# The low part of g in the dense layers: three of sixteen blocks made at another place in VectorE's order

## The chip, the core and the metric

The kernel runs on one core of a Trainium2 chip. The metric is the device time of one execution in microseconds. The engines are named as in the profile: PE (TensorE, matrix products; PEld is its weight loads), DVE (VectorE), ACT (ScalarE), POOL (GpSimd) and SP (SyncE, which issues DMAs here). Each works through its own list of instructions in order and waits on semaphores for the others.

## What is computed

Three parts in a row. Attention over 4 x 8 heads of 576 positions, once pooled by 4 and once in a narrow band; its output, reshaped, is x with 2304 tokens of 512 numbers. Two dense layers on x, which are the place of the change:

```python
h = x @ w_in                                  # 2304x512 @ 512x2048
g = np.where(h >= 1, h, np.where(h <= -1, 0.0, (h + 1) ** 2 / 4))
y = g @ w_out                                 # 2304x2048 @ 2048x512
```

Then a layer of 8 experts with a capacity of 288 tokens each, to which tokens are assigned by sorted gate logits.

## The kernel before

**Products in two parts.** To get fp32 precision, each operand is held as a high part, rounded to the type that PE multiplies, and a low part, the rest. A product is then three matmuls: high x high, high x low, low x high (`pe_halves`, line 528). For g the high part is a copy by ACT (line 640) and the low part a subtraction by DVE (line 669), which therefore has to wait for the copy.

**Chunks and steps.** The dense layers run over 9 chunks of 256 tokens, and each chunk over steps s = 0 to 18. The 2048 hidden features are 16 blocks f of 128. In step s PE makes the hidden block H(s) (12 matmuls, s below 16), and then adds block f = s - 3 to the output (6 matmuls of 512 columns, s from 3 on), for which it waits for the low part of g of that block (semaphore `glo_ready`). So there are three steps at the start with hidden products alone, and three at the end (16, 17, 18) with output products alone. The last chunk has no steps 16 to 18 on PE: after step 15 it takes blocks 13, 14 and 15 for the first half of the tokens and then for the second (`pe_last_products`).

**From H to g.** For block f DVE clamps H(f) to between -1 and 1 (line 660); ACT makes relu(H - 1) (line 633) and then squares the clamped one (line 634); DVE adds the two, which is g (line 665); ACT copies the high part (line 640); DVE subtracts for the low part (line 669). In DVE's list, step s holds the clamp of block s, the sum of block s - 1 and the low part of block s - 2. In ACT's list, step s holds relu and square of block s and the high part of block s - 1.

**What else stands in a step.** In step 0 PE turns the output of the chunk before for the gate logits, in step 1 it makes them, and DVE copies them out (line 556). In step 16 ACT and DVE split the next chunk's x into high (line 610) and low (line 615) parts, four pieces each; H(0) of the next chunk needs them piece by piece. Beside this runs the rest of the attention in units of two heads. Chunk 0 has a plan of its own with three units (`FIRST_PLAN`), chunks 1 to 4 have two units each (a loop), chunk 5 one, chunks 6 and 7 (a loop) and 8 none. A unit is spread over steps by `PLAN`: `turn` (PE turns q and k; ACT copies q; DVE copies k, line 372, and pools both over 4, lines 377 and 383), `scores`, two steps later the sums, `turn_p` (DVE copies a part of the turned probabilities, line 424) and `out` (PE makes the unit's output, lines 315 and 324; ACT copies its pooled part od, line 363; DVE adds both into xT, line 432). In chunks 1 to 4 `turn` of the first unit stands in step 1 and `out` of the second in step 16; in chunk 0 `turn_p` of its last unit stands in step 16 and `out` in 17. Chunk 0 also brings in the weights in pieces (ACT line 690, DVE line 707). POOL scales probabilities (lines 458, 465) and pools v.

In DVE's list the unit's instructions come last in a step, behind the instructions on g and the split of x.

```python
PLAN = [dict(turn=1, scores=3, turn_p=7, out=8), dict(turn=9, scores=11, turn_p=15, out=16)]
FIRST_PLAN = [dict(turn=None, scores=None, turn_p=1, out=2), dict(turn=3, scores=5, turn_p=9, out=10),
              dict(turn=11, scores=12, turn_p=16, out=17)]
```

Of the kernel before, what the change touches and what calls it, by code (L numbers as in the profile page):

```python
# [4 lines left out]
F32 = mybir.dt.float32  # L5
# [4 lines left out]
ALU = mybir.AluOpType  # L10
# [22 lines left out]
FC = FF // 128  # L33
# [3 lines left out]
RING = 4  # L37
# [29 lines left out]
def network(nc, q, k, v, w_in, w_out, w_gate, w1, w2, out, xt_dram, y_dram):  # L67
# [4 lines left out]
    with whole:  # L72
        def sem(name):
            return whole.enter_context(nc.semaphore(name))


        logits = whole.enter_context(nc.sbuf_tensor("logits", [128, YT + TILES, E], F32))
        ident = whole.enter_context(nc.sbuf_tensor("ident", [128, 128], F32))
        PS = whole.enter_context(nc.psum_tensor("PS", [128, 8, 512], F32))
        bank = [PS[:, i, :] for i in range(8)]  # L80

        con = {}
        for name, shape, dt in (("thr", [128, DIG, MOST], F32),
                                ("rev", [128, E], F32),
                                ("slot", [128, GP], F32),
                                ("weight", [128, DIG, TILES], F32),
                                ("three", [128, GT], F32),
                                ("tile_no", [128, TILES], F32),
                                ("part_no", [128, 1], F32),
                                ("alive", [128, TILES], F32),  # L90
                                ("zero", [128, TILES], F32),
                                ("unit", [128, DIG, 128], BF16),
                                ("below", [128, 128], BF16),
                                ("ones", [128, 128], BF16)):
            con[name] = whole.enter_context(nc.sbuf_tensor(name, shape, dt))
        made = sem("made")
        dense_layers(nc, sem, PS, bank, ident, logits, con, made, qf, kf, vf, w_in, w_out, w_gate, xt_dram, y_dram)
        experts(nc, sem, bank, ident, logits, con, made, w1, w2, y_dram, out)
# [8 lines left out]
def dense_layers(nc, sem, PS, bank, ident, logits, con, made, qf, kf, vf, w_in, w_out, w_gate, xt_dram, y_dram):  # L107

    ctx = ExitStack()
    with ctx:  # L110
        def sb(name, shape, dt=F32):
            return ctx.enter_context(nc.sbuf_tensor(name, shape, dt))
# [42 lines left out]
        c_sb = scratch[:, 3, 0:2 * CT].rearrange("p (a t) -> p a t", a=2)  # L155
        r_sb = scratch[:, 3, 2 * CT:4 * CT].rearrange("p (a t) -> p a t", a=2)
# [4 lines left out]
        g_sb = sb("g_sb", [128, 2, CT])  # L161
        g = [sb(f"g{s}", [128, RING, CT], F32R) for s in range(2)]
# [21 lines left out]
        h_ready, c_ready, r_ready, q_ready, g_ready = sem("h_ready"), sem("c_ready"), sem("r_ready"), sem("q_ready"), sem("g_ready")  # L184
        ghi_ready, glo_ready, g_used = sem("ghi_ready"), sem("glo_ready"), sem("g_used")
# [322 lines left out]
        def dve_units(dve, c, plan, s):  # L508
            for at, n, k, b in units_of(c, plan):
                if s == at["turn"]:  # L510
                    dve_kT(dve, n, TM)
                    dve_pool_k(dve, n)
                    dve_pool_q(dve, n)
                if s == at["scores"]:
                    dve_mask(dve, n, TM)
                    dve_dtop(dve, n, TM)
                if at["scores"] is not None and s == at["scores"] + 2:
                    dve_rden(dve, n, TM)
                    dve_rdend(dve, n)
                if s == at["turn_p"]:  # L520
                    dve_pT(dve, n, TM)
                if s == at["out"]:
                    dve_xT(dve, n, TM)
# [26 lines left out]
        def dve_yT(dve, c):  # L550
            dve.wait_ge(y_turned, YT * c + 2)
            dve.tensor_copy(yT[:, 1, :, :].rearrange("p k m -> p (k m)"), A[1][:, :]).then_inc(yT1_ready, 1)

        def dve_logits(dve, c):
            dve.wait_ge(lg_ready, c + 1)
            dve.tensor_copy(logits[:, ds(YT * c, YT), :].rearrange("p a e -> p (a e)"), A[2][:, 0:YT * E]).then_inc(lg_out, 1)
# [55 lines left out]
        def dve_split_x(dve, c):  # L612
            for kk in range(KC):
                dve.wait_ge(xs_hi, KC * c + kk + 1)
                dve.tensor_tensor(xs[1][:, kk, :], xload[:, kk, :], xs[0][:, kk, :].bitcast(F32),
                                  ALU.subtract).then_inc(xs_lo, 1)
# [9 lines left out]
        def act_chunk(act, c, units, first=False, more=True):  # L626
# [23 lines left out]
            act.wait_ge(y_stored, 16 * YT * c + 16)  # L650
            act.activation(y_sb[:, 0, :], Y[0][:, :], ACT.Copy).then_inc(y0_out, 1)

        def dve_chunk(dve, c, units, first=False, more=True):
            for s in range(STEPS):
                if first and s == FIRST_PLAN[0]["turn_p"]:
                    dve_units(dve, c, units, s)
                if s < FC:
                    dve.wait_ge(h_ready, FC * c + s + 1)
                    dve.wait_ge(g_ready, FC * c + s + 1)
                    dve.tensor_scalar(c_sb[:, s % 2, :], H[s % 2][:, 0:CT], -1.0, 1.0, ALU.max, ALU.min).then_inc(c_ready, 1)  # L660
                f = s - 1
                if 0 <= f < FC:
                    dve.wait_ge(q_ready, FC * c + f + 1)
                    dve.wait_ge(glo_ready, FC * c + f + 1)
                    dve.tensor_tensor(g_sb[:, f % 2, :], c_sb[:, f % 2, :], r_sb[:, f % 2, :], ALU.add).then_inc(g_ready, 1)  # L665
                f = s - 2
                if 0 <= f < FC:
                    dve.wait_ge(ghi_ready, FC * c + f + 1)
                    dve.tensor_tensor(g[1][:, f % RING, :], g_sb[:, f % 2, :], g[0][:, f % RING, :].bitcast(F32),  # L669
                                      ALU.subtract).then_inc(glo_ready, 1)  # L670
                if s == 0 and not first:
                    dve_yT(dve, c)
                if s == 1 and not first:
                    dve_logits(dve, c)
                if s == FC and more:
                    dve_split_x(dve, c + 1)
                if not first or s != FIRST_PLAN[0]["turn_p"]:
                    dve_units(dve, c, units, s)
                if first and s in CHUNK_PIECES:
                    dve_piece(dve, CHUNK_PIECES[s])  # L680
            dve.wait_ge(y_ready, YT * c + 2)
            dve.wait_ge(y_stored, 16 * YT * c + 16)
            dve.tensor_copy(y_sb[:, 1, :], Y[1][:, :]).then_inc(y1_out, 1)
# [20 lines left out]
        def dve_piece(dve, i):  # L704
            c = slice(ORDER[i] * PIECE, (ORDER[i] + 1) * PIECE)
            dve.wait_ge(piece_hi, i + 1)
            dve.tensor_tensor(W[1][:, c], scratch[:, SLOT_OF[i], :], W[0][:, c].bitcast(F32), ALU.subtract).then_inc(piece_lo, 1)

        with nc.Block() as block:  # L709
# [232 lines left out]
            def _(dve):  # L942
# [26 lines left out]
                dve_rdend(dve, EARLY)  # L969
                dve.wait_ge(mask_ready, 1)  # L970
                dve_chunk(dve, 0, FIRST_PLAN, first=True)
                with dve.Fori(1, MIXED) as c:
                    dve_chunk(dve, c, PLAN)
                dve_chunk(dve, MIXED, PLAN[0:1])
                dve.wait_ge(con_ready, 7)
                for i in range(1, DIG):
# [762 lines left out]
```

## Time and profile before

| | |
|---|---|
| time, median of 3 runs | 876.4 us (876.13, 876.4, 880.44) |
| profiled execution, first to last instruction | 876.4 us |
| PE busy | 825.6 us, 94% |
| PE weight loads | 747.9 us, 85% |
| DVE busy | 509.4 us, 58% |
| ACT busy | 406.7 us, 46% |
| POOL busy | 332.7 us, 38% |
| low part of g (DVE, line 669) | 144 instructions, 70.0 us |
| sum g (DVE, line 665) | 144 instructions, 63.0 us |
| high part of g (ACT, line 640) | 144 instructions, 58.5 us |

The attention's first units take the first 56 us, the dense layers (with the other units beside them) run from 56 to 569 us, and routing and experts from there to the end. The page's chain of work that ended last holds 34% of the span in all, and all its pieces lie behind 569 us. A busy PE is not a PE at its peak: its records overlap, so a delay shows both as idle time and as a longer group. In the timelines, a number in brackets is the idle time of the engine before that instruction and what ended it.

### The profile page before, as it was taken

The numbers are of one execution on the slowest core, as the hardware profiler recorded it, in microseconds if no ns is written. First come the engines' busy times: TensorE is split into PE (matmuls) and PEld (weight loads), VectorE is DVE, ScalarE is ACT, GpSimd is POOL, SyncE is SP. The second block draws the span as 40 slices with busy tenths as digits, with TensorE's granted clock in tenths as the row PEclk, the third lists the DMA queues.
The fourth block names the chain that finished last, engine by engine and source line by source line (L and its number), as shares of the span: only waits on it lengthen the run. The fifth ranks groups of instructions, "written<-read, shape, count | busy, mean of one in ns | idle before, by whom it ended". The sixth has DMA issues, their size and how long they took to land. (4 is left out here: it accounts for less than half of the span.)

```text
span 876.4 us, 21162 instructions
## 1 busy us (share of the span) xinstructions
PE 825.6 (94%) x7658; PEld 747.9 (85%) x7658; DVE 509.4 (58%) x1424; ACT 406.7 (46%) x1006; POOL 332.7 (38%) x391
## 2 busy tenths in 40 slices
PE   6979999999999999999999999939999999999995
PEld 4867888888888888888998989838999999999995
DVE  4668766655755665563434344376766766756620
ACT  4655555444534444553444444304455454454461
POOL 6661133203311331240000000007776786787782
PEclk9899999999999999999999999958999999999998
DMA  9975521321322223201101000005624625615511
GB/s 199 255 194 136 142 67 42 94 80 27 79 79 63 57 79 79 66 1 39 50 1 48 0 24 2 24 21 201 220 95 163 231 64 187 227 46 217 204 53 45
DMA packets 99301, 85.49 MB, mean 98 GB/s; under 512 B 63664, under 2 KB 71856, under 8 KB 99248
## 3 DMA queue, kind: packets, MB, share of 16 engines
q1 hardware_dynamic: 93808, 74.74, 29.7%
q0 software_dynamic: 3072, 9.44, 3.7%
q10 hardware_dynamic: 2368, 0.59, 0.4%
q8 instruction: 34, 0.56, 0.3%
q14 instruction: 19, 0.16, 0.1%
HBM read 70.60 MB, written 14.16 MB: 97 GB/s over the span
## 5 line engine op out<-in xcount | busy, mean ns | idle before, releaser
L528 PE MATMUL PS<-xs,W 128*128 128x256 f32 x1728 | 234.1, 285 | 1.3 <-DVE xT L432 1.3
L528 PEld LDWEIGHTS PS<-xs,W 128*128 128x128 f32 x1728 | 222.6, 189 | 12.4 <-issue 3.3
L528 PE MATMUL PS<-W,g 128*128 128x512 f32 x864 | 223.9, 396 | 5.3 <-DVE g L669 5.0
L528 PEld LDWEIGHTS PS<-W,g 128*128 128x128 f32 x864 | 152.5, 188 | 37.4 <-DVE g L669 9.7
L633 ACT ACTIVATE scratch<-PS,minus 128x256 f32<-128x256 f32 x144 | 68.1, 473 | 218.7 <-DVE scratch L660 218.7
L660 DVE TENSOR_SCALAR scratch<-PS 128x256 f32<-128x256 f32 x144 | 61.0, 423 | 124.4 <-PE PS L528 123.9
L441 POOL TENSOR_TENSOR P<-P,top 128x640 f32<-128x640 f32 x11 | 13.9, 1261 | 224.8 <-DVE top L391 224.8
L1539 POOL TENSOR_TENSOR w1s<-w1r,w1s 128x512 fp32r<-128x512 f32 x64 | 80.7, 1287 | 28.2 <-ACT w1s L1427 27.9
L1334 PE MATMUL PS<-exs,w1s 128*128 128x288 f32 x256 | 81.1, 317 | 0.0
L1334 PE MATMUL PS<-ehs,w2s 128*128 128x288 f32 x256 | 80.8, 316 | 0.0
L1335 PE MATMUL PS<-exs,w1s 128*128 128x288 f32 x256 | 76.0, 297 | 0.0
L1336 PE MATMUL PS<-exs,w1s 128*128 128x288 f32 x256 | 75.7, 296 | 0.0
L1335 PE MATMUL PS<-ehs,w2s 128*128 128x288 f32 x256 | 75.5, 295 | 0.0
L1336 PE MATMUL PS<-ehs,w2s 128*128 128x288 f32 x256 | 75.2, 294 | 0.0
L1571 POOL TENSOR_TENSOR w2s<-w2r,w2s 128x512 fp32r<-128x512 f32 x56 | 71.7, 1291 | 9.2 <-ACT w2s L1465 8.8
L634 ACT ACTIVATE scratch<-scratch,half 128x256 f32<-128x256 f32 x144 | 72.0, 500 | 0.0
L669 DVE TENSOR_TENSOR g<-g_sb,g 128x256 fp32r<-128x256 f32 x144 | 70.0, 486 | 0.1
L1616 POOL MEMSET full<- 128x8 bf16 x1 | 0.1, 109 | 178.0 <-POOLq L709 178.0
L665 DVE TENSOR_TENSOR g_sb<-scratch 128x256 f32<-128x256 f32 x144 | 63.0, 437 | 1.2 <-ACT scratch L634 1.1
L640 ACT ACTIVATE g<-g_sb 128x256 fp32r<-128x256 f32 x144 | 58.5, 407 | 1.4 <-DVE g_sb L665 1.4
L1461 ACT ACTIVATE ehs<-PS 128x288 fp32r<-128x288 f32 x64 | 26.3, 411 | 57.7 <-PE PS L1336 57.5
L1334 PEld LDWEIGHTS PS<-exs,w1s 128*128 128x128 f32 x256 | 48.9, 191 | 0.4
(198 smaller groups left out, 1433.3 us busy)
## 6 DMA issues: line engine op xcount, KB each, us to landing
w1r<-in_moe_w SPq DMA_DIRECT2D x16, 1024.0 KB, 5.1
w2r<-in_moe_w SPq DMA_DIRECT2D x16, 1024.0 KB
vd<-in_v SPq DMA_DIRECT2D x16, 288.0 KB
xt<-xT SPq DMA_DIRECT2D x16, 288.0 KB, 2.2
y<-scratch SPq DMA_DIRECT2D x18, 256.0 KB, 2.2
vw<-in_v SPq DMA_DIRECT2D x34, 128.0 KB, 2.8
scratch<-in_moe_w_in SPq DMA_DIRECT2D x8, 512.0 KB, 5.9
scratch<-in_moe_w_out SPq DMA_DIRECT2D x8, 512.0 KB, 4.8
```

Of the source, the lines that this page charges most:

```text
L528: r = pe.matmul(psum, wsel(w[i]), xsel(x[j]), start=first and t == 0, stop=last and t == 2)
L633: act.activation(r_sb[:, s % 2, :], H[s % 2][:, 0:CT], ACT.Relu, bias=minus[:, :]).then_inc(r_ready, 1)
L634: act.activation(c_sb[:, s % 2, :], c_sb[:, s % 2, :], ACT.Square, bias=half[:, :], scale=0.5).then_inc(q_ready, 1)
L640: act.activation(g[0][:, f % RING, :], g_sb[:, f % 2, :], ACT.Copy).then_inc(ghi_ready, 1)
L660: dve.tensor_scalar(c_sb[:, s % 2, :], H[s % 2][:, 0:CT], -1.0, 1.0, ALU.max, ALU.min).then_inc(c_ready, 1)
L665: dve.tensor_tensor(g_sb[:, f % 2, :], c_sb[:, f % 2, :], r_sb[:, f % 2, :], ALU.add).then_inc(g_ready, 1)
L669: dve.tensor_tensor(g[1][:, f % RING, :], g_sb[:, f % 2, :], g[0][:, f % RING, :].bitcast(F32), ALU.subtract).then_inc(glo_ready, 1)
L1334: pe.matmul(psum, wh, xh, start=first, stop=False)
L1335: pe.matmul(psum, wh, xl, start=False, stop=False)
L1336: return pe.matmul(psum, wl, xh, start=False, stop=last)
L1539: pool.tensor_tensor(w1s[1][:, :, c], w1r[:, :, c], w1s[0][:, :, c].bitcast(F32), ALU.subtract).then_inc(w1_lo, 1)
L1571: pool.tensor_tensor(w2s[1][:, f, :], w2r[:, f, :], w2s[0][:, f, :].bitcast(F32), ALU.subtract).then_inc(w2_lo, 1)
```

## The change

The sum and the low part of g become two small functions, `dve_g` and `dve_g_rest`, with the waits that they had. In DVE's list three of the sixteen low parts of each chunk stand elsewhere:

- block 0: in step 1, behind the sum of block 0 and the copy of the logits, ahead of the unit's instructions of that step (before: in step 2, behind the sum of block 1);
- block 14: in step 16, now ahead of the sum of block 15 (before: right behind it);
- block 15: in step 16, behind the sum of block 15 and ahead of the split of x and of the unit's instructions (before: in step 17).

The other thirteen, and the lists of the other engines, are as before; no instruction is added or taken away.

```diff
--- before.py
+++ after.py
@@ -650,6 +650,16 @@
             act.wait_ge(y_stored, 16 * YT * c + 16)
             act.activation(y_sb[:, 0, :], Y[0][:, :], ACT.Copy).then_inc(y0_out, 1)
 
+        def dve_g(dve, c, f):
+            dve.wait_ge(q_ready, FC * c + f + 1)
+            dve.wait_ge(glo_ready, FC * c + f + 1)
+            dve.tensor_tensor(g_sb[:, f % 2, :], c_sb[:, f % 2, :], r_sb[:, f % 2, :], ALU.add).then_inc(g_ready, 1)
+
+        def dve_g_rest(dve, c, f):
+            dve.wait_ge(ghi_ready, FC * c + f + 1)
+            dve.tensor_tensor(g[1][:, f % RING, :], g_sb[:, f % 2, :], g[0][:, f % RING, :].bitcast(F32),
+                              ALU.subtract).then_inc(glo_ready, 1)
+
         def dve_chunk(dve, c, units, first=False, more=True):
             for s in range(STEPS):
                 if first and s == FIRST_PLAN[0]["turn_p"]:
@@ -658,20 +668,20 @@
                     dve.wait_ge(h_ready, FC * c + s + 1)
                     dve.wait_ge(g_ready, FC * c + s + 1)
                     dve.tensor_scalar(c_sb[:, s % 2, :], H[s % 2][:, 0:CT], -1.0, 1.0, ALU.max, ALU.min).then_inc(c_ready, 1)
-                f = s - 1
-                if 0 <= f < FC:
-                    dve.wait_ge(q_ready, FC * c + f + 1)
-                    dve.wait_ge(glo_ready, FC * c + f + 1)
-                    dve.tensor_tensor(g_sb[:, f % 2, :], c_sb[:, f % 2, :], r_sb[:, f % 2, :], ALU.add).then_inc(g_ready, 1)
-                f = s - 2
-                if 0 <= f < FC:
-                    dve.wait_ge(ghi_ready, FC * c + f + 1)
-                    dve.tensor_tensor(g[1][:, f % RING, :], g_sb[:, f % 2, :], g[0][:, f % RING, :].bitcast(F32),
-                                      ALU.subtract).then_inc(glo_ready, 1)
+                if s == FC:
+                    dve_g_rest(dve, c, FC - 2)
+                if 1 <= s <= FC:
+                    dve_g(dve, c, s - 1)
+                if s == FC:
+                    dve_g_rest(dve, c, FC - 1)
+                if 3 <= s < FC:
+                    dve_g_rest(dve, c, s - 2)
                 if s == 0 and not first:
                     dve_yT(dve, c)
                 if s == 1 and not first:
                     dve_logits(dve, c)
+                if s == 1:
+                    dve_g_rest(dve, c, 0)
                 if s == FC and more:
                     dve_split_x(dve, c + 1)
                 if not first or s != FIRST_PLAN[0]["turn_p"]:
```

## Rows read from the trace of the kernel before

A row of a timeline gives start (us), length (us), engine, line and operation, output and inputs, and the number of instructions merged into it. A row of waits gives the engine and line that waited, what released it, and then total, count and longest.

**Rows 1.** Busy time by stretch; then granted TensorE clock, DMA share, GB/s

```profile
56.00:566.00 510.00, 502.08 (x4180) 446.23 (x4180) 288.43 (x685) 243.99 (x645) 87.34 (x140) 1.00 0.21 58
600.00:606.00 6.00, 6.00 (x48) 5.92 (x47) 2.78 (x8) 1.54 (x5) 6.00 (x6) 0.55 0.86 298
```

**Rows 2.** Waits of PE over the span: total us, times, longest us

```profile
PE PS L528 <- DVE g L669: 5.0, 11, 1.2
```

**Rows 3.** Timeline of PE, two undisturbed steps of a chunk: start us, length us

```profile
484.75 1.59 PE L528 MATMUL PS<-xs,W 128*128 128x256 f32 x12
486.18 1.54 PE L528 MATMUL PS<-W,g 128*128 128x512 f32 x6
487.56 1.59 PE L528 MATMUL PS<-xs,W 128*128 128x256 f32 x12
```

**Rows 4.** Timeline of PE, first block of chunk 4

```profile
312.19 3.12 PE L528 MATMUL PS<-xs,W 128*128 128x256 f32 x24
315.71 1.67 PE L528 MATMUL PS<-W,g 128*128 128x512 f32 x6 [0.39 <-DVE g L669]
```

**Rows 5.** Timeline of all engines at 310 us, start of chunk 4

```profile
310.84 0.41 ACT L640 ACTIVATE g<-g_sb 128x256 fp32r<-128x256 f32 x1
...
311.40 0.17 DVE L556 COPY logits<-PS 128x16 f32 x1 [1.04 <-PE PS L543]
...
312.45 0.76 DVE L372 COPY kT<-PS 128x576 f32<-128x576 f32 x1 [0.87 <-PE PS L249]
```

**Rows 6.** Timeline of all engines at 299 us, end of chunk 3, with a unit's output

```profile
299.69 0.41 ACT L640 ACTIVATE g<-g_sb 128x256 fp32r<-128x256 f32 x1
...
300.44 1.43 DVE L615 TENSOR_TENSOR xs<-scratch,xs 128x256 fp32r<-128x256 f32 x4 [0.74 <-ACT xs L610]
...
302.42 3.42 PE L528 MATMUL PS<-W,g 128*128 128x512 f32 x12
...
303.70 0.42 DVE L669 TENSOR_TENSOR g<-g_sb,g 128x256 fp32r<-128x256 f32 x1
```

**Rows 7.** Timeline of all engines at 464 us, end of chunk 6, without units

```profile
463.15 4.37 PE L528 MATMUL PS<-W,g 128*128 128x512 f32 x18
...
464.71 0.43 DVE L665 TENSOR_TENSOR g_sb<-scratch 128x256 f32<-128x256 f32 x1 [0.27 <-ACT scratch L634]
465.05 0.42 DVE L669 TENSOR_TENSOR g<-g_sb,g 128x256 fp32r<-128x256 f32 x1
465.25 0.42 ACT L640 ACTIVATE g<-g_sb 128x256 fp32r<-128x256 f32 x1 [0.26 <-DVE g_sb L665]
...
466.01 1.43 DVE L615 TENSOR_TENSOR xs<-scratch,xs 128x256 fp32r<-128x256 f32 x4 [0.54 <-ACT xs L610]
...
467.83 1.66 PE L528 MATMUL PS<-W,g 128*128 128x512 f32 x6 [0.31 <-DVE g L669]
```

**Rows 8.** Timeline of all engines at 561 us, end of the last chunk

```profile
561.30 0.42 DVE L665 TENSOR_TENSOR g_sb<-scratch 128x256 f32<-128x256 f32 x1 [0.27 <-ACT scratch L634]
561.64 0.99 DVE L669 TENSOR_TENSOR g<-g_sb,g 128x256 fp32r<-128x256 f32 x2
...
562.11 3.28 PEld L528 LDWEIGHTS PS<-W,g 128*128 128x128 f32 x15 [0.50 <-DVE g L669]
```

**Rows 9.** Timeline of all engines at 70 us, start of chunk 0

```profile
70.32 0.82 DVE L432 TENSOR_TENSOR xT<-PS,od 128x348 f32<-128x348 f32 x2 [0.76 <-ACT od L363]
```

**Rows 10.** Timeline of all engines at 117 us, end of chunk 0

```profile
116.70 1.65 POOL L465 TENSOR_TENSOR Pd<-Pd,rdend 72x288 f32<-72x288 f32 x2
116.94 0.88 DVE L669 TENSOR_TENSOR g<-g_sb,g 128x256 fp32r<-128x256 f32 x1
...
119.55 0.41 DVE L424 COPY pT<-PS 128x256 f32<-128x256 f32 x1
...
120.63 1.37 PE L315 MATMUL PS<-pT,vw 64*64 64x58 f32 x40
```

**Rows 11.** Timeline of PE, first products of chunk 0

```profile
56.21 4.50 PE L528 MATMUL PS<-xs,W 128*128 128x256 f32 x24 [1.30 <-DVE xT L432]
```

## The prediction

> **What bounds the kernel now.** I read four views, in this order. Busy time by stretch: between 56 and 566 us, the dense layers, PE is busy for 502.1 of 510 us at a granted clock of 1.00 (2.4 GHz), DVE for 288 [rows 1]. So in this stage only what makes PE wait counts, and there are 8 us of PE idle to win at all. The chain that ended last is of no use here: it reaches back only to the routing, behind the dense stage. The waits of PE: of that idle, 5.0 us in 11 pieces end with the low part of g (line 669), the longest 1.2 [rows 2]. Then the timelines around those pieces. The reader should see in them the order in which DVE works, for each of the waits ends with an instruction that DVE could have run earlier.
>
> How to price one piece. An undisturbed step is 12 hidden products (from 484.75 to 486.18, 1.43 us) and 6 output products (to 487.56, 1.38 us); a group starts 0.16 us before the one ahead of it has ended, and six output products take 1.54 us [rows 3]. So an idle of i shown on PE is a delay of i + 0.16, and the group behind a wait is longer (1.67 for 1.54), since its first weight load was not done ahead [rows 4]. A piece costs **i + 0.29 us**.
>
> **Term 1, the first block (f = 0), five chunks with units (1 to 5).** The low part of g for f = 0 was made in step 2, behind the unit's copy of kT and both poolings: PE, which ended H(2) and H(3) at 315.31, starts the output products at 315.71, idle 0.39, released by it [rows 4]. Now it is made in step 1, behind the logits copy and ahead of kT. Its input, the high part, is done at 310.84 + 0.41 = 311.25, before the logits copy starts (311.40), and DVE sits idle from 311.57 to 312.45, until PE has turned k [rows 5]. An instruction of 0.42 us fits there with some 0.4 to spare: the move costs nothing, and the wait it adds (on the high part) is already met; behind it on DVE stand kT and the poolings, with PE's scores behind those, but not even they move. If that cover were gone, kT, the poolings and clamp(2) would come 0.34 later (the next instruction starts that long after one of these, 465.05 behind 464.71 [rows 7]). The output products of f = 0 then follow H(3) at once. What is late next is PE itself. Gain: 5 x (0.39 + 0.29) = **3.4 us**. The three chunks without units show no such wait and gain nothing here.
>
> **Term 2, the last block (f = 15), four chunks (1 to 4) that end with a unit's output.** Step 17 makes the low part of f = 15 at 303.70, behind the split of x and behind xT, and xT waits for ScalarE's copy of od. PE shows no idle but a stretched group: 12 output products take 3.42 us, where 1.67 + 1.38 = 3.05 would do [rows 3, 4, 6]. Now DVE makes it as soon as ScalarE has the high part, 299.69 + 0.41 = 300.10, some 3.5 us sooner. g(15) comes one instruction later (0.34), but ScalarE is at pdT until 299.7 and picks it up hardly later; the split starts at about 300.5 instead of 300.44, and xT waits for od until 302.96 anyway [rows 6]. Gain: 4 x 0.37 = **1.5 us**.
>
> **Term 3, the last block, three chunks (5 to 7) without a unit at the end.** There g(15) ran at 464.71 and the low part of f = 14 at 465.05, right when its high part came. The new order puts g(15) behind that: 465.05 + 0.34 = 465.39, 0.68 later. ScalarE starts the high part of f = 15 0.54 behind g(15): 465.93, done 466.35; the low part runs from 466.40 to 466.82, and the wait it adds for that high part is where DVE idles, some 0.7 us, with the split behind it. PE wants it at about 467.36, 0.16 before the end of its group (463.15 + 4.37 = 467.52), so 0.5 us are to spare, where today it starts at 467.83 [rows 7]. The split, behind it, ends near 468.1 instead of 467.44; H(0) of the next chunk needs its first quarter at 468.7 and the last one 1.1 us later. Gain: 3 x (0.31 + 0.29) = **1.8 us**. The count fits: 5 + 3 pieces here and in term 1 make 2.9 us of idle, and the other 3 of the 11, with 2.1 us and the longest, are in chunk 0 at blocks that the change does not move [rows 2].
>
> **Term 4, the last chunk, a loss.** With no H left and the products ordered by token tile, PE takes f = 13, 14, 15 with three products each, so that it wants f = 15 at 562.11 + 0.13 + 3 x 0.23 = 562.93. Today the low part of f = 15 ends at 561.64 + 0.99 = 562.63 and no one waits for it. Now g(15) waits for the low part of f = 14 (which can't start before 561.64): 561.98 instead of 561.30. ScalarE starts 0.54 behind it, ends at 562.94, the low part ends at 563.40, and PE starts at 563.45: 0.52 + 0.13, **0.6 us lost** [rows 7, 8]. The move that wins in term 3 loses here, since PE comes one and a half groups sooner.
>
> **Term 5, chunk 0.** At its start the low part of f = 0 is no longer in step 2, but what PE does behind that block, the turn of the next unit, waits for xT, which ends at 71.14 and depends on PE and ScalarE alone: 0 [rows 9]. At its end a unit's turn_p falls into step 16, so now pT's copy on DVE (119.55 to 119.96) comes behind the wait for the high part of f = 15. POOL works until 118.35, and DVE's two-input subtraction beside it takes 0.88 instead of 0.42 [rows 10]. With slow ones: low(14) to about 117.5, g(15) to 118.3, low(15) from 118.8, split to 120.4, pT to 120.8; PE, which starts the unit's output at 120.63, would wait 0.2 us. With none slow it waits 0; with every one of the seven instructions 0.46 longer than the quick ones, near 1.0. I take the slow rows that stand there: **0.3 us lost**, bounds 0 and 1.0.
> The Trainium skill, GPSIMD Engine Reference, section Key points, says that GpSimd shares its SBUF interfaces with VectorE and that they contend when the DVE instruction has two SBUF inputs; that speaks against queueing three such instructions in a row ahead of the split. The trace agrees where POOL runs (0.88 for 0.42), and by the rule as by the row the sum is the same as long as POOL rests at the ends of chunks 1 to 8.
>
> **Sum.** -3.4 - 1.5 - 1.8 + 0.6 + 0.3 = -5.8 us. The profiled execution spans 876.4 us and the median of the runs is 876.4, so the sum is made against both alike: **870.6 us**. No instruction, byte or DMA is added, and SP's and POOL's queues keep their order. Everything behind the dense stage moves forward as a block. A measurement of this kernel can tell about 0.5%, 4.4 us, from no change.
>
> **Rivals.**
> A. As computed: 870.6, own range 869.5 to 872.0. Chance 0.63.
> B. The gains are partly given back: the waits move on to the next thing that DVE or ScalarE owes (r of a block, P of a unit through POOL). For it speaks that five of the gains come right ahead of a unit's scores; against it, that DVE is busy for only 288 of the 510 us [rows 1]. With term 1 halved and term 2 lost: 870.6 + 1.7 + 1.5 = 873.8. Chance 0.15.
> C. The clock at the start of the experts. At 600 to 606 us the granted clock is 0.55, though PE is busy throughout [rows 1]. The dense stage ends sooner, so the stretch can lie otherwise over the first expert products. Its price from rows: 24 hidden products took 4.50 us at 56 us, begun at the lower level (1.2 GHz), and 3.12 at the higher one, a difference of 1.4 [rows 4, 11]. Either sign: 872.0 (chance 0.07) or 869.2 (0.05).
> D. It does not do what it says: PE is held by its own sequencer behind these semaphores and the gaps stay; terms 4 and 5 remain: 876.4 + 0.9 = 877.3. Chance 0.04. Against it: line 669 at 303.70 ends at 304.12, inside the stretched group [rows 6].
> E. Slower: the split of x becomes what ends last. From low(14) to the last quarter there are seven two-input instructions; if POOL ran beside all, each took 0.46 longer, 3.2 us in all, against a slack of 1.7 (468.1 against 468.7 + 1.1). It decides from a delay of 1.7 us on. Over by 1.5 us at the eight chunk ends ahead of another chunk it costs 12 us: 882.6; it takes four such ends to use up the 5.8. For it speaks the slow row in chunk 0 [rows 10]; against it, that POOL has no units left at the ends of chunks 5 to 7. Chance 0.06.
>
> **How the numbers follow.** The likeliest is A. Faster by over 0.5% (below 872.0): A but its tail, half of C: 0.66. Within: B, D, the rest of A and C: 0.28. Slower: E: 0.06. The range takes in A, C and B: 869.1 to 874.6.
>
> **What would show it.** After the change PE's waits on line 669 fall from 11 to about 4 (three in chunk 0, one or two in the last chunk); the groups behind H(3) in chunks 1 to 5 start 0.16 before its end; the 12 products at a chunk's end take 3.05; the last chunk shows a new wait of about 0.4; pT of chunk 0 ends near 120.8. Wrong would be: a wait of PE for the split of x, or a later kT copy.

## The result, and the profile after

| | before | after |
|---|---|---|
| median of 6 runs each | 877.1 us (875.7 to 880.4) | 873.1 us (872.4 to 875.4) |
| ratio after / before, 95% interval | | 0.9943 [0.9922, 0.9964] |
| profiled execution | 876.4 us | 873.6 us |

The change makes the kernel 0.57% faster, 5.0 us of 877, with an interval from 3.2 to 6.8 us. The ratio is not that of the two medians, which lie 4.0 us apart. Forecast were 5.8 us. The interval holds it, and the measured median lies within the forecast range of 869.1 to 874.6.

The waits of PE for the low part of g went from 5.0 us in 11 pieces [rows 2] to this (line 660 is now the low part, 656 the sum), in the view of waits of PE of the kernel after: total, count, longest.

```profile
PE PS L528 <- DVE g L660: 1.5, 4, 0.6
```

Not all of that fall is the change's. Three of the pieces lie in chunk 0, at blocks that the change does not move: they add up to 2.2 us before and to 1.2 here, where 8.2 us of chunk 0 ran at half clock (the granted clock at 0.5, 1.2 GHz) instead of 3.1. When the same kernel ran again (e0_again below) they were 2.2 again, and all waits for the low part 2.5 us in 4 pieces.

In the view of busy time by stretch, PE idles 5.4 of the 510 us between 56 and 566 us, where it idled 7.9 [rows 1]; the granted clock is 0.99. The dense stage ends at 562.1 now (565.9 before), so the last 4 us of this window belong to what follows it.

```profile
56.00:566.00 510.00, 504.59 (x4208) 451.53 (x4204) 291.39 (x689) 245.74 (x648) 87.30 (x143) 0.99 0.21 59
```

What follows is the same place as in rows 4 and 5, the start of chunk 4, in the timeline of all engines of the kernel after. The high part (line 640) is done at 310.34, the low part runs at 310.60 between the logits copy and kT, and the copy of kT waits for PE as before. The output products start at 314.26, 0.16 before the hidden ones end (311.30 + 3.12), with no wait, and take 1.55 instead of 1.67.

```profile
309.94 0.40 ACT L640 ACTIVATE g<-g_sb 128x256 fp32r<-128x256 f32 x1
...
310.51 0.17 DVE L556 COPY logits<-PS 128x16 f32 x1 [1.04 <-PE PS L543]
310.60 0.41 DVE L660 TENSOR_TENSOR g<-g_sb,g 128x256 fp32r<-128x256 f32 x1
...
311.30 3.12 PE L528 MATMUL PS<-xs,W 128*128 128x256 f32 x24
311.56 0.76 DVE L372 COPY kT<-PS 128x576 f32<-128x576 f32 x1 [0.54 <-PE PS L249]
...
314.26 1.55 PE L528 MATMUL PS<-W,g 128*128 128x512 f32 x6
```

The end of chunk 3, as in rows 6: the low part of block 15 is ahead of the split, the split starts 0.34 behind it, and twelve output products take 3.04 us, where it was 3.42.

```profile
299.28 0.42 ACT L640 ACTIVATE g<-g_sb 128x256 fp32r<-128x256 f32 x1
...
299.73 0.43 DVE L660 TENSOR_TENSOR g<-g_sb,g 128x256 fp32r<-128x256 f32 x1 [0.56 <-ACT g L640]
...
300.07 1.43 DVE L615 TENSOR_TENSOR xs<-scratch,xs 128x256 fp32r<-128x256 f32 x4
...
301.88 3.04 PE L528 MATMUL PS<-W,g 128*128 128x512 f32 x12
```

The end of chunk 6, as in rows 7. The low part of block 14 at 461.86, then the sum of block 15, ACT's high part 0.53 later, the low part of block 15 at 463.18, the split. PE goes on without a wait.

```profile
461.42 0.40 ACT L640 ACTIVATE g<-g_sb 128x256 fp32r<-128x256 f32 x1
461.86 0.42 DVE L660 TENSOR_TENSOR g<-g_sb,g 128x256 fp32r<-128x256 f32 x1 [0.57 <-ACT g L640]
462.20 0.42 DVE L656 TENSOR_TENSOR g_sb<-scratch 128x256 f32<-128x256 f32 x1
462.73 0.42 ACT L640 ACTIVATE g<-g_sb 128x256 fp32r<-128x256 f32 x1 [0.91 <-DVE g_sb L656]
...
463.18 0.43 DVE L660 TENSOR_TENSOR g<-g_sb,g 128x256 fp32r<-128x256 f32 x1 [0.56 <-ACT g L640]
463.52 1.42 DVE L615 TENSOR_TENSOR xs<-scratch,xs 128x256 fp32r<-128x256 f32 x4
...
465.58 1.59 PE L528 MATMUL PS<-xs,W 128*128 128x256 f32 x12
```

The end of the last chunk, as in rows 8. Here the same order leaves PE idle at 559.10, until the low part that began at 558.62 has ended.

```profile
557.38 0.42 DVE L660 TENSOR_TENSOR g<-g_sb,g 128x256 fp32r<-128x256 f32 x1 [0.58 <-ACT g L640]
557.72 0.42 DVE L656 TENSOR_TENSOR g_sb<-scratch 128x256 f32<-128x256 f32 x1
...
558.17 0.42 ACT L640 ACTIVATE g<-g_sb 128x256 fp32r<-128x256 f32 x1 [0.83 <-DVE g_sb L656]
558.62 0.43 DVE L660 TENSOR_TENSOR g<-g_sb,g 128x256 fp32r<-128x256 f32 x1 [0.48 <-ACT g L640]
...
559.10 2.12 PE L528 MATMUL PS<-W,g 128*128 128x512 f32 x8 [0.27 <-DVE g L660]
```

And the end of chunk 0, as in rows 10. The sum, beside POOL, takes 0.89, but the low part of block 14 ahead of it takes 0.43, and the split is as quick as elsewhere (1.42 for four), and pT's copy ends at 122.50, in time for the unit's output.

```profile
119.03 0.89 DVE L656 TENSOR_TENSOR g_sb<-scratch 128x256 f32<-128x256 f32 x1
...
120.75 1.42 DVE L615 TENSOR_TENSOR xs<-scratch,xs 128x256 fp32r<-128x256 f32 x4
...
122.09 0.41 DVE L424 COPY pT<-PS 128x256 f32<-128x256 f32 x1
...
122.76 1.37 PE L315 MATMUL PS<-pT,vw 64*64 64x58 f32 x40
```

**Where the time went.** One number per chunk says more than the total. It is the time from the first hidden product of a chunk to that of the next (in the last, to the last output product), read from the starts of line 528 in the timeline.

| us | ahead | 0 | 1 | 2 | 3 | 4 | 5 | 6 | 7 | 8 | behind |
|---|---|---|---|---|---|---|---|---|---|---|---|
| before | 56.2 | 67.87 | 60.56 | 60.53 | 60.51 | 60.53 | 54.76 | 48.36 | 48.30 | 47.80 | 310.9 |
| after | 58.2 | 68.00 | 59.50 | 59.55 | 59.51 | 59.55 | 53.59 | 47.68 | 47.75 | 48.41 | 311.9 |
| after less before | +2.0 | +0.1 | -1.1 | -1.0 | -1.0 | -1.0 | -1.2 | -0.7 | -0.6 | +0.6 | +1.0 |

The nine chunks are 5.7 us shorter. The two stretches around them, whose instructions the change does not touch, are 3.0 longer in this pair of executions, which is why the profiled executions differ by 2.8 us alone. The 2.0 ahead go with the clock: between 0 and 56 us the granted clock is 0.91 before and 0.85 after. In the four of the 14 profiled executions where it is 0.85 to 0.87, the stretch ahead takes 58.2 to 59.6 us; in the ten with 0.88 or more, 56.0 to 57.1. Behind the dense layers both have some 32 us at half clock (32.1 and 32.3), so the 1.0 there does not come from more time at half clock; its cause is open.

### The profile page after: what moved, and what is told of

It is laid out like the page before. It is cut to its first block and busy times, and to the rows that moved or that the text cites. A ratio compares the mean times of both kernels' runs of the same rounds, so it can differ in the third digit from the quotient of the medians.

```text
span 873.6 us, 21162 instructions
## 1 busy us (share of the span) xinstructions
PE 827.0 (95%) x7658; PEld 752.3 (86%) x7658; DVE 509.8 (58%) x1424; ACT 406.9 (47%) x1006; POOL 332.5 (38%) x391
## 5 line engine op out<-in xcount | busy, mean ns | idle before, releaser
L528 PE MATMUL PS<-W,g 128*128 128x512 f32 x864 | 221.4, 394 | 1.5 <-DVE g L660 1.5
```

The costliest lines, as they stand in the source:

```text
L528: r = pe.matmul(psum, wsel(w[i]), xsel(x[j]), start=first and t == 0, stop=last and t == 2)
```

## The experiments

Theory: PE's waits for the low part of g came from VectorE's order alone, and each goes where VectorE gets there earlier. Rivals: B, the gain is given back at the next wait; E, the split of x becomes late. Chunks 1 to 8 repeat to within 0.1 us between executions, so I read them from the trace, and use timed runs for the total. Ratios are to the kernel before on the same chip, in the same session; e4, e5, e6, e10 and e11 have one profiled execution each and no ratio. The diffs are against the changed kernel, where nothing else is said.

| run | 0 | 1 | 2 | 3 | 4 | 5 | 6 | 7 | 8 | sum 1 to 8 | behind |
|---|---|---|---|---|---|---|---|---|---|---|---|
| e0_again | 67.92 | 59.49 | 59.50 | 59.50 | 59.50 | 53.51 | 47.75 | 47.74 | 48.39 | 435.4 | 307.6 |
| e1_first_only | 67.84 | 59.87 | 59.85 | 59.85 | 59.85 | 54.08 | 48.29 | 48.33 | 47.87 | 438.0 | 306.7 |
| e4_behind_turn | 67.97 | 59.91 | 59.91 | 59.85 | 59.86 | 54.09 | 48.29 | 48.32 | 47.86 | 438.1 | 309.8 |
| e2_last_only | 68.25 | 60.19 | 60.20 | 60.20 | 60.20 | 54.25 | 47.71 | 47.70 | 48.32 | 438.8 | 308.2 |
| e3_keep14 | 67.97 | 59.55 | 59.55 | 59.51 | 59.55 | 53.51 | 47.76 | 47.75 | 47.88 | 435.1 | 306.4 |
| e8_swap | 68.02 | 59.49 | 59.50 | 59.50 | 59.50 | 53.52 | 47.71 | 47.75 | 47.88 | 434.8 | 314.3 |
| e5_pad4 | 68.05 | 59.85 | 59.84 | 59.83 | 59.83 | 53.91 | 48.31 | 48.13 | 48.74 | 438.4 | 312.4 |
| e10_pad4_end | 68.79 | 59.50 | 59.50 | 59.50 | 59.55 | 53.63 | 47.99 | 47.75 | 48.38 | 435.8 | 306.8 |
| e6_pad9 | 69.29 | 59.60 | 59.60 | 59.60 | 59.60 | 54.41 | 50.81 | 48.88 | 48.51 | 441.0 | 311.5 |
| e11_pad9_end | 67.91 | 59.52 | 59.55 | 59.51 | 59.55 | 54.43 | 49.25 | 48.84 | 48.43 | 439.1 | 309.5 |
| e7_shift_g | 68.05 | 59.85 | 59.84 | 59.84 | 59.84 | 53.90 | 48.11 | 48.12 | 48.74 | 438.2 | 306.4 |
| e9_shift_xs | 68.34 | 59.60 | 59.60 | 59.60 | 59.60 | 53.70 | 47.99 | 48.01 | 48.15 | 436.2 | 307.2 |

### The changed kernel again

> The changed kernel once more, beside the others of this series. The nine chunks (from the first hidden product of one to that of the next) took 67.9, 60.6, 60.5, 60.5, 60.5, 54.8, 48.4, 48.3, 47.8 us before and 68.0, 59.5, 59.5, 59.5, 59.5, 53.6, 47.7, 47.8, 48.4 after. Theory (the gain lies in the order of VectorE): chunks 1 to 8 repeat to 0.05 us each, sum 435.5 against 441.4; what else differs between runs lies ahead of the dense layers, in chunk 0 and in the experts, and follows the granted clock. Rival (part of the gain is given back behind the dense layers): the stretch behind them is again about 1 us longer than before.

Ratio 0.9947 [0.9933, 0.9961], 870.2 against 875.6 us. Chunks 1 to 8 repeat within 0.08 us each. Behind them it takes 307.6 us, 3.3 less than in the profiled execution of before. That alone does not show that nothing is given back there, for the runs were made on several chips, and this stretch differs by chip: from the first product of the third expert to that of the seventh, one expert takes 33.2 to 33.3 us in the four runs on chip 0 (e0 to e3), 33.3 to 33.4 in the four on chip 11 (e7, e9, e10, e11) and 33.8 in the four on chip 13 (e4, e5, e6, e8), with the same instructions. It took 33.8 in both profiles of the first pair. What speaks to it are the timed ratios, which compare on one chip. Over the eight kernels that have one (the first result, e0, e1, e2, e3, e7, e8, e9) the timed gain is 4.4 us on average and the nine chunks are 4.7 us shorter. In seven of them the chunks' gain lies inside the timed interval, and for this run it stands at the edge (5.9 in the chunks, 3.4 to 5.9 by the ratio). So nothing like the 3.2 us of rival B is given back; a few tenths can't be excluded.

### Block 0 alone

```diff
-                if s == FC:
-                    dve_g_rest(dve, c, FC - 2)
                 if 1 <= s <= FC:
                     dve_g(dve, c, s - 1)
-                if s == FC:
-                    dve_g_rest(dve, c, FC - 1)
-                if 3 <= s < FC:
+                if 3 <= s <= FC + 1:
                     dve_g_rest(dve, c, s - 2)
```

> Only block 0's low part is moved to step 1; blocks 14 and 15 are as before. Theory: chunks 1 to 5 get shorter by 0.66 each, 3.3 us in all, chunks 6 to 8 stay at 48.4, 48.3, 47.8; the total falls by 3.3 us. Rival B (given back): the wait moves on to the unit's scores or to the next low part and less than 0.3 per chunk is left, 1.7 in all or less.

Ratio 0.9957 [0.9943, 0.9972]. Chunks 1 to 5 are shorter by 0.69, 0.68, 0.66, 0.68 and 0.68, 3.4 us in all; 6 to 8 are as before. Rival B would have left less than 0.3 each. It falls for this term.

### Blocks 14 and 15 alone

```diff
-                if 3 <= s < FC:
+                if 2 <= s < FC:
                     dve_g_rest(dve, c, s - 2)
...
-                if s == 1:
-                    dve_g_rest(dve, c, 0)
```

> Only blocks 14 and 15 are moved in step 16; block 0 is as before, in step 2. Theory: chunks 1 to 4 shorter by 0.35 each, 5 to 7 by 0.5 to 0.6 each, 8 longer by 0.6, chunk 0 by 0 to 0.3: together 2.5 us less. Rival B: the next chunk starts no sooner, since its hidden products then wait for the split of x, and nothing is gained in chunks 5 to 7.

Ratio 0.9977 [0.9961, 0.9993]. Chunks 1 to 4 are shorter by 0.37, 0.33, 0.31, 0.33 (1.3 us), 5 to 7 by 0.51, 0.65, 0.60 (1.8 us), and 8 is longer by 0.52. The two halves of the change add up: 3.4 and 2.6 against 6.0 for the whole (e0_again) in chunks 1 to 8.

### Block 14 left behind the sum of block 15

```diff
-                if s == FC:
-                    dve_g_rest(dve, c, FC - 2)
                 if 1 <= s <= FC:
                     dve_g(dve, c, s - 1)
+                if 3 <= s <= FC:
+                    dve_g_rest(dve, c, s - 2)
                 if s == FC:
                     dve_g_rest(dve, c, FC - 1)
-                if 3 <= s < FC:
-                    dve_g_rest(dve, c, s - 2)
```

> As the changed kernel, but in step 16 the low part of block 14 stays behind the sum of block 15; only block 15's is moved ahead of the split of x. Theory: the wait that the changed kernel has in the last chunk comes only from block 14 standing ahead of the sum, so chunk 8 falls back from 48.4 to 47.8, and all others stay at 59.5 (1 to 4), 53.6, 47.7, 47.8; 0.6 us less than the changed kernel in all. Rival (the two low parts in a row are what delays it): chunk 8 stays at 48.4.

Chunk 8 falls to 47.88, the others stay. In the timeline of all engines of this kernel the sum is back at 0.34 ahead of the low part of block 14, both low parts (x2) have ended at 559.35, and PE's products wait for none of them. What is left is the wait of the weight loads (PEld) for block 14, 0.50 as before the change [rows 8]; the changed kernel had 0.47 there and another 0.71 for block 15.

```profile
558.02 0.43 DVE L656 TENSOR_TENSOR g_sb<-scratch 128x256 f32<-128x256 f32 x1 [0.27 <-ACT scratch L634]
558.36 0.99 DVE L660 TENSOR_TENSOR g<-g_sb,g 128x256 fp32r<-128x256 f32 x2
558.48 0.42 ACT L640 ACTIVATE g<-g_sb 128x256 fp32r<-128x256 f32 x1 [0.18 <-DVE g_sb L656]
558.84 3.30 PEld L528 LDWEIGHTS PS<-W,g 128*128 128x128 f32 x15 [0.50 <-DVE g L660]
```

So the loss in the last chunk came from block 14 standing ahead of the sum, and no chunk needs it there. By its trace this version beats both kernels, by 0.5 us over the changed one in chunk 8; its ratio of 0.9932 [0.9911, 0.9953] overlaps with the 0.9947 of the changed one, so timing alone doesn't tell them apart.

### Block 0 in step 1, but behind the unit

```diff
-                if s == 1:
-                    dve_g_rest(dve, c, 0)
...
                 if not first or s != FIRST_PLAN[0]["turn_p"]:
                     dve_units(dve, c, units, s)
+                if s == 1:
+                    dve_g_rest(dve, c, 0)
```

(and blocks 14 and 15 as before)

> Only block 0's low part is moved to step 1, but to its end, behind the unit's copy of kT and the poolings. Theory (PE waited only since the low part stood behind clamp(2) and the sum of block 1, about 0.7 us of VectorE's work): it then ends at about 315.0 on the time base of before, ahead of H(3)'s end at 315.3, and chunks 1 to 5 get shorter by 0.66 each, as with the place ahead of the unit. Rival (the place ahead of the poolings is what matters): at most half of it, 0.3 each. In chunk 0 it stands ahead of the weight piece as in the other.

Chunks 1 to 5 are as with the place ahead of the unit, to 0.06 us. The timeline of all engines of this kernel, start of chunk 4, shows why: the low part at 313.44, ahead of the clamp, ends 0.3 us before the hidden products (311.06 + 3.11 = 314.17), and the output products follow at once.

```profile
311.06 3.11 PE L528 MATMUL PS<-xs,W 128*128 128x256 f32 x24
...
313.44 0.42 DVE L660 TENSOR_TENSOR g<-g_sb,g 128x256 fp32r<-128x256 f32 x1
313.77 0.42 DVE L670 TENSOR_SCALAR scratch<-PS 128x256 f32<-128x256 f32 x1
...
314.02 1.55 PE L528 MATMUL PS<-W,g 128*128 128x512 f32 x6
```

What PE had waited for were the clamp and the sum that stood ahead of it, 0.7 us, not the poolings. The place ahead of the poolings is free, but it isn't what brings the gain.

### How late may the split of x be?

One instruction more on VectorE between the low part of block 15 and the split, in chunks 1 to 7:

```diff
                 if s == FC:
                     dve_g_rest(dve, c, FC - 1)
+                    if more and not first:
+                        dve.tensor_reduce(spare[:, :], g_sb[:, 0:1, :].to_broadcast([128, 4, CT]), AX.X, ALU.add)
```

with 9 in the place of 4 in the second pair. In e5 and e6 `spare` was allocated ahead of g, in e10 and e11 behind g.

> The changed kernel with one more instruction on VectorE between the low part of block 15 and the split of x in chunks 1 to 7: a sum over 4 x 256 elements, about 1.1 us, whose result nobody uses. It asks for the slack of the split. After the change the first piece of the split ends at 463.94 and PE takes it at 465.35 in chunk 6, 1.4 us of slack. Theory: nothing is lost, chunks 5 to 7 stay at 53.6, 47.7, 47.8. Rival E (the split ends last from a small delay on): they get longer by up to 1.1 each.

> The same with 9 x 256 elements, about 2.5 us. Theory: at the ends of chunks 5 to 7 the split is then late by 2.5 - 1.4 = 1.1 and the restart adds 0.1, so each gets longer by 1.1 to 1.3 us; chunks 1 to 4, where PE has a unit's output to make before, stay at 59.5 (slack there some 3.5 us). Rival E would have 2.5 each in all seven; no effect at all would mean that the hidden products do not hang on it.

e5 was a miss: every chunk from 1 to 8 was longer by 0.3 to 0.6 us than in e0_again, the last one too, which has no such instruction. A late split can't do that. But the output products came every 0.2334 us instead of 0.2291. The new tensor of 4 numbers ahead of g had moved g by 32 bytes. In e6 the shift was 64 bytes, the pace 0.2301, and the chunks behind the late splits were longer, but in chunk 6 by more than a late split explains (below). Hence both again at the old address:

> As the run with the sum over 4 x 256 elements ahead of the split of x, but the unused result lies behind all other tensors, so that g starts at the same SBUF address as in the changed kernel. In the first try, where it lay ahead of g and moved it by 32 bytes, the output products came every 0.2334 us instead of 0.2291, which made all chunks longer. Theory: at the old address the pace is 0.2291 again and the inserted 1.1 us costs nothing: chunks 59.5 (1 to 4), 53.6, 47.7, 47.7, 48.4. Rival (VectorE's extra instruction itself slows PE): 59.8, 53.9, 48.3, 48.1, 48.7 as in the first try.

> The same for the sum over 9 x 256 elements, 2.5 us. Theory: the split is late by 2.5 - 1.4 = 1.1 us at the ends of chunks 5, 6 and 7 alone; these get longer by 1.1 to 1.3 us each (the next chunk's first product comes later) and chunks 1 to 4 stay at 59.5. A stretch at half clock behind such a wait, as the first try showed one behind chunk 5, would come on top.

e10: 1.1 us more ahead of the split cost nothing measurable in chunks 1 to 4, 7 and 8, and 0.12 in chunk 5. Chunk 6 has 0.24 more. Half of it lies at its gate logits, whose 16 products take 1.95 us instead of the 1.85 of e0_again; the other half I have no cause for. Chunk 0, which has no such instruction, has 0.9 more, with a stretch of 6.8 us at half clock near its start. e11: chunks 1 to 4 stay, 5 to 7 are longer by 0.92, 1.50 and 1.10, 3.5 us in all. In its timeline of all engines, end of chunk 5, the inserted sum takes 2.55 us, the split starts at 417.04, 2.46 behind it, and PE waits for it, idle 0.64 (plus the overlap of 0.16 and the unprefetched start).

```profile
414.23 0.43 DVE L661 TENSOR_TENSOR g<-g_sb,g 128x256 fp32r<-128x256 f32 x1 [0.48 <-ACT g L641]
414.58 2.55 DVE L679 TENSOR_REDUCE spare<-g_sb 128x9 f32<-128x2304 f32 x1
...
417.04 1.42 DVE L616 TENSOR_TENSOR xs<-scratch,xs 128x256 fp32r<-128x256 f32 x4
...
417.51 1.70 PE L529 MATMUL PS<-xs,W 128*128 128x256 f32 x12 [0.64 <-DVE xs L616]
```

So the slack of the split at these ends lies between 1.1 and 2.5 us. The waits for it at the ends of chunks 5, 6 and 7 are 0.64, 0.61 and 0.80 us. Priced as before (plus 0.29) that is 0.9, 0.9 and 1.1 lost, and the slack is 2.46 - 0.64 - 0.16, some 1.7 us (1.5 at the end of chunk 7), not the 1.4 of the expectation. The rest of chunk 6's 1.50 is a second wait that the late split brings with it: at 421.81 the gate logits' products wait 0.29 us for ACT's copy (line 549), which they do not in e0_again. Rival E's mechanism is real, but the change is 1.5 us or more away from it.

### The address of g alone

```diff
+        shift = sb("shift", [128, 8])
         g = [sb(f"g{s}", [128, RING, CT], F32R) for s in range(2)]
```

> The changed kernel with 32 unused bytes ahead of the two tensors of g, and nothing else: they start at 220832 and 224928 instead of 220800 and 224896, a multiple of 32 but not of 64. Theory of the address: output products every 0.2334 instead of 0.2291 us, 96 of them in a chunk, 0.3 to 0.4 us longer per chunk and 3 us in all. Rival (the first try's slower pace came with its extra instruction or was that execution's own): 0.2291 and the chunks of the changed kernel.

Ratio 0.9973 [0.9954, 0.9991], where the changed kernel without the shift had 0.9947 [0.9933, 0.9961]; the intervals overlap, so the chunks have to tell. Chunks 1 to 8 add up to 438.2 against 435.4. The view of groups by line, of the changed kernel again and of this one: 864 output products, busy time and mean.

```profile
L528 PE MATMUL PS<-W,g 128*128 128x512 f32 x864 | 221.3, 394 | 2.5 <-DVE g L660 2.5
```

```profile
L529 PE MATMUL PS<-W,g 128*128 128x512 f32 x864 | 224.2, 397 | 2.5 <-DVE g L661 2.5
```

Their start to start is 0.2333 us. So the address is shown as the cause of e5's miss; what in the memory makes it so is not. The same with x, in the version with block 14 left in its place (e3_keep14):

```diff
+        shift = sb("shift", [128, 8])
         xs = [sb(f"xs{s}", [128, KC, CT], F32R) for s in range(2)]
...
+        shift_g = sb("shift_g", [128, 8])
         g = [sb(f"g{s}", [128, RING, CT], F32R) for s in range(2)]
```

> The version that keeps block 14 behind the sum of block 15, with the two parts of x moved by 32 bytes from 210464 to 210496, from a multiple of 32 to one of 64, and g by 64 bytes, which keeps it a multiple of 64. If the address of what PE streams or loads matters for its pace, the hidden products may come faster than every 0.1195 us (1728 of them: 0.001 each is 1.7 us). Rival: no difference; chunks 59.5, 53.5, 47.75, 47.75, 47.9 as without the shift.

The hidden products came every 0.1193 instead of 0.1196 us, but the output products every 0.2317 instead of 0.2293; chunks 1 to 8 take 436.2 against the 435.1 of e3_keep14. Ratio 0.9941 [0.9922, 0.9960]. Nothing was won with these two shifts together; x alone was not moved. "A multiple of 64" is not the rule either, since g stood on one here. It is not g's address alone, for in e6_pad9 g stood at the same one (64 bytes on) and the pace was 0.2301. What differed there was the place of x, the order of block 14 and the inserted sum.

### Chunk 0: the low part ahead of the sum where PE waits

Against e3_keep14:

```diff
+                swapped = first and s in (4, 6, 15)
+                if swapped:
+                    dve_g_rest(dve, c, s - 2)
                 if 1 <= s <= FC:
                     dve_g(dve, c, s - 1)
-                if 3 <= s <= FC:
+                if 3 <= s <= FC and not swapped:
                     dve_g_rest(dve, c, s - 2)
```

> As the version that keeps block 14 behind the sum of block 15, and in chunk 0, steps 4, 6 and 15, the low part of the earlier block stands ahead of the sum of the later one. These are the three steps of chunk 0 where PE waited for a low part before and still waits (0.2 to 1.2 us idle each). Theory: each of these waits shrinks by 0.34 us, chunk 0 by up to 1.0 us (less where its start runs at half clock), the others as in the version without it: 47.8 in chunk 8, total 0.6 to 1.6 us under the changed kernel. Rival (the sum's delay pushes ScalarE's high part, which makes the next low part late): chunk 0 does not get shorter.

A miss: chunk 0 took 68.02 us, no less than without it (67.97). Ratio 0.9924 [0.9905, 0.9943], not to be told from 0.9932. In its timeline of PE two of the three waits for the low part are gone, and one is 0.33:

```profile
77.92 1.63 PE L528 MATMUL PS<-W,g 128*128 128x512 f32 x6 [0.33 <-DVE g L660]
...
85.22 1.62 PE L528 MATMUL PS<-W,g 128*128 128x512 f32 x6
...
93.46 0.77 PE L300 MATMUL PS<-ident,Pd 72*72 72x72 f32 x8 [0.46 <-POOL Pd L465]
...
118.49 0.77 PE L300 MATMUL PS<-ident,Pd 72*72 72x72 f32 x8 [0.21 <-POOL Pd L465]
```

The one at 77.92 did not shrink: it was 0.26 in e3_keep14. The other two were 0.36 and 0.61, and in their place PE now idles 0.46 and 0.21 us for POOL's scaling of Pd (line 465) at the turn of the probabilities. Both executions had 6.8 us of chunk 0 at half clock. So rival B holds in chunk 0: there the unit's work that ends on POOL is the next to be late, and an earlier low part only moves the wait. This is one execution of each; chunk 0 differs by 0.5 us between most executions.

## Why the prediction was right

- **Term 1** (first block, 5 x 0.68 = 3.4): 3.4 with that part alone. The wait that it adds on DVE was met in advance, as said. The pricing rule, idle + 0.29, is what made it right: the idle time shown was 0.39, the chunk got 0.68 shorter. The prediction put the copy of kT and both poolings in front of the late low part; e4_behind_turn shows that only the clamp and the sum, which also stood there, mattered.
- **Term 2** (four ends with a unit's output, 1.5): 1.3. The stretched group, 3.42, became 3.04.
- **Term 3** (three ends without, 1.8): 1.8. DVE's times, moved 0.68 for the sum and 0.54 to the high part, came out at 0.34 + 0.53 behind the low part of block 14.
- **Term 4** (the last chunk, +0.6): +0.6 in the changed kernel and its repetition, +0.5 in e2_last_only. The loss was in the forecast and its cause is shown: with block 14 left in its place it is gone.
- **Term 5** (chunk 0, +0.3, bounds 0 and 1.0) was mis-sized. At its end PE's unit output starts 1.62 us behind the group ahead of it (121.14 to 122.76) where it was 1.56 (119.07 to 120.63): 0.06 us. The step that failed is which instructions run slow beside POOL. I had put both the low part of block 14 and the sum there. But the low part of 14, now ahead of the sum, started at 118.69, ahead of POOL's scaling of Pd (118.77), and took 0.43. Only the sum, which started behind POOL's, was slow (0.89). The next low part, at 120.41, was quick again (0.42); POOL ended at 120.45.
- **Sum**: -5.8 forecast, -5.7 in the nine chunks of the profiled pair, -5.0 [-6.8, -3.2] in the timed runs. The step that the sum left out is what lies around the dense layers. I took it to move as a block; in 14 profiled executions it took 56.0 to 59.6 us ahead and 306.4 to 314.3 behind, with the same instructions. That is more than the whole change. A part of it goes with the clock (ahead) and with the chip (behind), as shown above. That the forecast 870.6 and the measured 873.1 lie so close is in part luck: 0.7 us of the 2.5 is before's own median (877.1 in the end), and the other 1.8 is 5.8 forecast against 4.0 between the medians, within this spread.
- **Rivals.** B is refuted for chunks 1 to 8 and true for chunk 0. D falls with the waits. E needs 1.5 us or more beyond what the change puts ahead of the split. C could not be tested by itself: where the half-clock stretches lie can't be set. In the profiled pair it did not come about: the time at half clock behind the dense layers was 32.1 us before and 32.3 after.

## What to carry to other kernels

Where PE is at its limit, look in front of each of its idle pieces for the last instruction of the engine that released it, and ask what stood ahead of that in its queue which nobody was waiting for; price the piece with the lost overlap and the unprefetched start, not by the idle time alone. A new order is right only for a given arrival time of the consumer: the last round of a loop, with another order of products, wanted the same block earlier and lost what the others won. And when the effect is half a per cent, measure it in the stretches that contain it, and leave the addresses of all tensors alone.

## What the runs showed of the hardware that I had not expected

- Moving two tensors by 32 bytes in SBUF changed the start to start of the products that load their weights from them from 0.2291 to 0.2333 us (e0_again and e7_shift_g), 2.8 us in chunks 1 to 8, half of what the change brings.
- Once, half clock came behind waits in the dense layers. In e6_pad9 PE waited 0.67 us for the split ahead of 418.16 and 0.29 more (for ACT) at 422.46, and the 24 hidden products from 424.27 took 4.60 us instead of 3.12; the view of busy time by stretch gives the granted clock (third number from the end) as 0.72 there, though PE was busy throughout, so a part of it ran at 1.2 GHz. e11_pad9_end, with the same inserted time, had waits of 0.64 and 0.29 at the same places and no such stretch, so whether the waits brought it is not shown.

```profile
418.16 1.70 PE L529 MATMUL PS<-xs,W 128*128 128x256 f32 x12 [0.67 <-DVE xs L616]
...
424.27 4.60 PE L529 MATMUL PS<-xs,W 128*128 128x256 f32 x24
```

```profile
418.00:424.00 6.00, 5.54 (x46) 5.34 (x46) 4.37 (x19) 2.53 (x6) 0.00 (x0) 1.00 0.54 177
424.00:430.00 6.00, 6.00 (x34) 5.79 (x34) 2.35 (x7) 1.81 (x5) 0.00 (x0) 0.72 0.00 2
430.00:436.00 6.00, 6.00 (x41) 5.46 (x40) 2.18 (x6) 2.72 (x8) 0.00 (x0) 1.00 0.00 0
```

- The pace of the experts differs by chip: 33.8 us for one expert in the four runs on chip 13 and 33.2 to 33.4 in the eight on chips 0 and 11, as given at e0_again.
- In chunk 0 half clock cost little. Its length was 67.8 to 68.3 us in 12 of 14 executions, with 3.1 to 8.2 us of it at half clock. PE waited less for VectorE in some of these: ahead of block 2, 0.24 us in the kernel after (8.2 us at half clock) and 1.19 in its repetition (3.4). It is not the amount alone, for e4_behind_turn had 3.5 us, begun 8.4 us into the chunk, and the same 0.24. Only e10_pad4_end, with 6.8 us in one stretch, and e6_pad9, with 10.2 us, took 68.8 and 69.3.
